# Eight of the fourteen slots of the second MLP's down-layer weights combined beside the first MLP

## The chip, the cores and the metric

The kernel runs on one core of a Trainium2 chip. The metric is the device time of one execution in microseconds, the median of several runs. The engines are named as in the profile: PE is TensorE, PEld its weight loads, DVE is VectorE, ACT is ScalarE, POOL is GpSimd and SP is SyncE, which issues all DMAs of this kernel.

## The reference

A linear attention with an RMS norm gives x of 8 batches, 576 tokens and 512 features. Two blocks follow, each with an MLP of 2048 hidden features:

```python
X = np.fft.fft(np.fft.fft(x, axis=1), axis=2)
u = x + np.real(X)
un = (u - mu) / np.sqrt(var + 1e-06)
x = u + np.maximum(un @ w_ch1, 0.0) @ w_ch2          # first MLP, weights moe_*

u = x + ((x.transpose(0, 2, 1) @ U) @ V).transpose(0, 2, 1)
out = u + np.maximum(u @ w_ch1, 0.0) @ w_ch2         # second MLP, weights moe2_*
```

All is fp32, and the kernel must keep nearly all of that precision.

## The kernel before

**Stages.** Attention and the Fourier transform take the first 280 us. Then come 12 rounds (`g` in the code, `NG`), each of 768 tokens: rounds 0 to 5 are the first MLP, rounds 6 to 11 (`g >= NS`, `NS` = 6) the second. Each layer is a Strassen product: the 2 x 2 blocks of tokens and weights are combined into 7 products (1 to 7), for which sums or differences of blocks are needed on both sides. Each operand is split into a high and a low part (fp32r), and PE computes high*high, high*low and low*high.

**Steps.** A round has 56 steps (`t`), 28 of the up layer (lines L838 to L840) and 28 of the down layer (L855 to L857), each of 12 matmuls of 384 columns. "Down half" is steps 28 to 55. The down products go in the order `DN_ORDER` = (2, 5, 1, 4, 3, 7, 6), four steps each. For each down step DVE makes the low part `t_lo` (`lo_dn`, L1332), and for products of two blocks it or, for every fourth step, POOL first adds the blocks of h (`raw_dn`: L1351 on DVE, L1556 on POOL); ACT makes the high part (`hi_dn`, L1068 and L1074). There are five buffers of these entries, so an entry is made at most five steps ahead. DVE also takes finished products out of PSUM: `d5` (L1377) at its place 36, `d1` (L1381) at 40, and so on. In the second MLP, after `d1`, POOL adds a block twice (`add_first`, L1566).

**Weights.** Two steps share a slot of weights, so a round has 28 slots (14 up, 14 down) that go through a ring of 7 buffers of 1 MB (`RING`). A slot is either loaded ready, combined and split, from the scratch tensors `wc1` and `wc2` (L515), or made from the raw weights ("raw slot"): SP loads one or two blocks (L509), POOL adds them if there are two (`sum_slot`, L1542, 8 steps ahead of the use), ACT makes the high part (`split_slot_hi`, L987, 7 ahead), DVE the low part (`split_slot_lo`, L1266, 6 ahead), and SP stores the result to `wc2` for the rounds that follow (`store_w`, L526). In rounds 0 and 6 all 14 down slots are raw. Products 3 and 4 take one block and need no sum.

**Up pieces.** The combined up weights of the second MLP are made in rounds 1 to 4 already: eight units go through the buffer `pb_v`, two in a round: load at step 2 or 30, five small sums on POOL 4 steps later, ACT 7 later, DVE 8 later (L1260), and two stores.

**Orders by hand.** Each engine walks through all rounds and steps in a fixed order, with semaphore waits; what is listed at step t runs when the engine gets there. Rounds 1 to 6 have, between the steps of the up half, the turning of the last round's result (PE L722), its sum (DVE L1405) and split (`split_x2_lo`, DVE L1410, which writes `x_lo`), and a gather product (PE L752 to L754, at steps 4, 7, ..., 19) that waits for `x_lo`. Rounds 5 and 6 mix the second block's input in (L764, DVE L1421).

Of the kernel before, what the change touches and what calls it, by code (L numbers as in the profile page):

```python
# [166 lines left out]
def build_program(nc, k_main, k_rest, v_main, v_rest, q_t, g_norm, wr1a, wr2a, wr1b, wr2b, u_perm, v_perm,  # L169
# [114 lines left out]
    with ExitStack() as ctx:  # L284
# [12 lines left out]
        def sem(name):  # L297
# [38 lines left out]
        PB = {"0": (pb[0], pb_raw[0]), "1": (pb[1], pb_raw[1]), "v": (pb_v, pb_v_raw)}  # L336
        UNITS = [("01"[f % 2], f // 2, 0, f) for f in range(8)] + [("v", f, 1, f) for f in range(8)]
        UNIT_AT = {(1 + f // 2, 2 + 28 * (f % 2)): UNITS[8 + f] for f in range(8)}

        def stored_units(mlp, h):  # L340

# [3 lines left out]
                    need[name] = max(need.get(name, 0), n + 1)  # L345
            return need

        def slot_sum(r, i):

            high, low = w_raw[r][:, 0, :, :, :], w_raw[r][:, 1, :, :, :]  # L350
# [47 lines left out]
        def _(sp):  # L398
# [9 lines left out]
            def load_unit(unit):  # L408
                name, n, mlp, f = unit
                if n:  # L410
                    sp.wait_ge(p_stored[name], 32 * n)
                sp.dma_start(PB[name][1][:, 0, 0:4, :], wr[mlp][0][:, f // 4, :, f % 4].rearrange("b p c -> p b c")).then_inc(
                    p_loaded[name], 16)

            def store_unit(unit):
                name, n, mlp, f = unit
                sp.wait_ge(p_lo[name], n + 1)
                for part in range(2):
                    sp.dma_start(wc1[mlp][:, f // 4, :, part, f % 4].rearrange("i p c -> p i c"),
                                 PB[name][0][:, part, :, :].bitcast(F32)).then_inc(p_stored[name], 16)  # L420
# [68 lines left out]
            def load_w(n):  # L489

                r, mlp = n % RING, n // NSLOT // NS
                layer = n % NSLOT // len(UP_SLOTS)
                i, h = slot_product(n)
                if n >= RING:

                    sp.wait_ge(step, 2 * (n - RING) + 2)
                    if stored_slot(n - RING):
                        sp.wait_ge(w_stored[r], 16 * stores_of(n - RING))
                if raw_slot(n):
                    blocks = wr[mlp][layer][:, h].rearrange("b p f c -> b p (f c)")  # L500
                    names = {1: (0, 3), 2: (2, 3), 3: (0,), 4: (3,), 5: (0, 1), 6: (0, 2), 7: (1, 3)}[i]
# [59 lines left out]
            for g in range(NG):  # L561
                for j in range(NSLOT):
# [354 lines left out]
        def _(act):  # L917
# [56 lines left out]
            def split_unit_hi(unit):  # L974
# [169 lines left out]
            for g in range(NG):  # L1144
                more = g < NG - 1
                for t in range(NSTEP):
# [42 lines left out]
                            deviation(3 * (g + 1) + LN_AT.index(t - 1))  # L1189
                    if (g, t - 7) in UNIT_AT:  # L1190
                        split_unit_hi(UNIT_AT[g, t - 7])
                    for n in RAW_SLOTS:
                        if NSTEP * g + t == max(0, 2 * n - 7):
                            split_slot_hi(n)

        @block.vector
        def _(dve):
# [237 lines left out]
            for g in range(NG):  # L1435
                more = g < NG - 1
                for t in range(NSTEP):
# [65 lines left out]
        def _(pool):  # L1503
# [21 lines left out]
            def sum_unit(unit):  # L1525
# [8 lines left out]
                nc.gpsimd.tensor_tensor(raw[:, 1, 3, :], a21, a11, ALU.subtract)  # L1534
                nc.gpsimd.tensor_tensor(raw[:, 1, 4, :], a12, a22, ALU.subtract).then_inc(p_summed[name], 1)

            def sum_slot(n):

                r = n % RING
                pool.wait_ge(w_loaded[r], 16 * (n // RING + 1))  # L1540
                x, y, op = slot_sum(r, slot_product(n)[0])
# [46 lines left out]
            for g in range(NG):  # L1588
                more = g < NG - 1
                for t in range(NSTEP):  # L1590
# [94 lines left out]
```

## Time and profile before

| | |
|---|---|
| median of 3 runs | 1872.03 us (1871.91 to 1872.23) |
| the profiled execution | 1872.23 us, of which 1869.9 us from first to last instruction |
| granted TensorE clock, mean | 0.973 |
| PE busy | 1758.9 us, 94% |
| DVE busy | 1376.1 us, 74% |
| ACT busy | 783.4 us, 42% |
| POOL busy | 601.4 us, 32% |
| DMA | 470.04 MB, 251 GB/s on the mean |

A stretch in which PE's busy time falls behind the stretch's length is one where something else sets the time; which one is read from the wait before its matmuls. The bounds of the stretches below are the first up and down matmuls of the rounds: round 3's down half begins at 762.2 us, round 5 at 951.4, its down half at 1020.2, round 6 at 1082.3, its down half at 1153.1, round 7 at 1233.6 and its down half at 1299.9.

### The profile page before, as it was taken

What the parts mean: (1) busy time and instruction counts of PE and PEld (TensorE: products, weight loads), DVE (VectorE), ACT (ScalarE), POOL (GpSimd) and SP (SyncE); (2) the same over time, 40 slices, a digit from 0 to 9 for tenths busy, and PEclk for the clock granted to TensorE, in tenths of its full rate; (3) what the DMA queues carried; (4) which work ended last, traced back from release to release, by engine and by line L of the source; (5) the groups of instructions that cost most, each with busy time, mean ns of one, the idle gap of its engine ahead of it and who ended that gap; (6) DMA issues with size and microseconds to landing.
All of it is one profiled execution on the core that took longest, in us unless ns stands there. A gap on an engine that the chain in (4) does not pass through costs nothing.

```text
span 1869.9 us, 25843 instructions
## 1 busy us (share of the span) xinstructions
PE 1758.9 (94%) x9908; PEld 1691.3 (90%) x9908; DVE 1376.1 (74%) x1559; ACT 783.4 (42%) x1126; POOL 601.4 (32%) x428
## 2 busy tenths in 40 slices
PE   5989878889999999999999999799999999999998
PEld 5777758879999999999999999789999999999998
DVE  4787875997786787777866768965856947758667
ACT  1333333634544544444444436334335434443442
POOL 2777873453042131240320213620410402303203
PEclk9989879989999999999999999899999999999999
DMA  7457548888788688787876678786766666766663
GB/s 250 160 200 233 189 163 295 304 325 308 254 293 287 247 286 286 264 301 256 296 261 239 241 252 308 284 306 221 240 240 240 233 240 248 248 222 238 229 248 121
DMA packets 123819, 470.04 MB, mean 251 GB/s; under 512 B 12273, under 2 KB 49649, under 8 KB 84018
## 3 DMA queue, kind: packets, MB, share of 16 engines
q1 hardware_dynamic: 123698, 468.39, 71.5%
q8 instruction: 81, 1.33, 0.3%
q14 instruction: 40, 0.33, 0.1%
HBM read 389.70 MB, written 78.64 MB: 250 GB/s over the span
## 4 chain that ended last, share of the span: by engine, by line
PE 71%; DVE 11%; POOL 8%; issue 5%; DMA 3%; SPq 1%; ACT 0%; DVEq 0%; POOLq 0%; ACTq 0%
PE pair L838 11%; PE pair L840 11%; PE pair L839 11%; PE pair L855 11%; PE pair L857 10%; PE pair L856 10%; DVE t_raw L1351 3%; DVE t_lo L1332 2%; PE tr_ps L722 2%; DMA in_sb<-x_dram 1%; POOL x_sb L1520 1%; POOL x_sb L1511 1%; DMA q_sb<-q_t 1%; POOL w_raw L1542 1%; POOL x_sb L1519 1%
## 5 line engine op out<-in xcount | busy, mean ns | idle before, releaser
L855 PE MATMUL pair<-t_hi,w_sb 128*128 128x384 f32 x1344 | 463.1, 345 | 32.1 <-DVE t_lo L1332 31.9
L838 PE MATMUL pair<-t_hi,w_sb 128*128 128x384 f32 x1344 | 460.8, 343 | 17.3 <-DVE h_sb L1369 9.2
L856 PE MATMUL pair<-t_lo,w_sb 128*128 128x384 f32 x1344 | 458.8, 341 | 0.0
L857 PE MATMUL pair<-t_hi,w_sb 128*128 128x384 f32 x1344 | 458.5, 341 | 0.0
L839 PE MATMUL pair<-t_lo,w_sb 128*128 128x384 f32 x1344 | 455.8, 339 | 0.0
L840 PE MATMUL pair<-t_hi,w_sb 128*128 128x384 f32 x1344 | 455.6, 339 | 0.0
L1332 DVE TENSOR_TENSOR t_lo<-t_raw,t_hi 128x768 fp32r<-128x768 f32 x300 | 349.0, 1171 | 17.1 <-ACT t_hi L1059 13.7
L1556 POOL TENSOR_TENSOR t_raw<-h_sb 128x768 f32<-128x768 f32 x60 | 150.3, 2504 | 574.1 <-PE pair L857 574.1
L1074 ACT ACTIVATE t_hi<-t_raw 128x768 fp32r<-128x768 f32 x240 | 202.1, 846 | 314.2 <-DVE t_raw L1351 236.1
L855 PEld LDWEIGHTS pair<-t_hi,w_sb 128*128 128x128 f32 x1344 | 255.0, 190 | 41.1 <-DVE t_lo L1332 40.8
L838 PEld LDWEIGHTS pair<-t_hi,w_sb 128*128 128x128 f32 x1344 | 252.8, 188 | 24.5 <-issue 19.7
L839 PEld LDWEIGHTS pair<-t_lo,w_sb 128*128 128x128 f32 x1344 | 252.9, 188 | 3.0
L856 PEld LDWEIGHTS pair<-t_lo,w_sb 128*128 128x128 f32 x1344 | 255.0, 190 | 0.3
L857 PEld LDWEIGHTS pair<-t_hi,w_sb 128*128 128x128 f32 x1344 | 255.0, 190 | 0.0
L840 PEld LDWEIGHTS pair<-t_hi,w_sb 128*128 128x128 f32 x1344 | 252.8, 188 | 0.0
L1556 POOL TENSOR_TENSOR t_raw<-a_sb 128x768 f32<-128x768 f32 x60 | 124.9, 2085 | 322.6 <-PE pair L840 283.8
L1351 DVE TENSOR_TENSOR t_raw<-h_sb 128x768 f32<-128x768 f32 x180 | 206.4, 1147 | 20.0 <-PE pair L857 20.0
L1332 DVE TENSOR_TENSOR t_lo<-h_sb,t_hi 128x768 fp32r<-128x768 f32 x96 | 96.3, 1016 | 23.4 <-ACT t_hi L1068 23.4
L1266 DVE TENSOR_TENSOR w_sb<-w_raw,w_sb 128x1024 fp32r<-128x1024 f32 x76 | 109.7, 1443 | 0.6 <-ACT w_sb L987 0.6
L1373 DVE TENSOR_TENSOR h_sb<-pair,h_sb 128x768 f32<-128x768 f32 x48 | 46.0, 958 | 84.7 <-PE pair L840 84.6
L1511 POOL TENSOR_TENSOR x_sb<-x_sb,gn_sb 96x256 f32<-96x256 f32 x96 | 78.2, 845 | 84.1 <-DVE x_sb L1214 84.1
L1364 DVE TENSOR_TENSOR h_sb<-pair,h_sb 128x768 f32<-128x768 f32 x48 | 46.0, 958 | 68.3 <-PE pair L840 68.3
(149 smaller groups left out, 2120.9 us busy)
## 6 DMA issues: line engine op xcount, KB each, us to landing
w_sb<-wc SPq DMA_DIRECT2D x260, 1024.0 KB, 4.9
wc<-w_sb SPq DMA_DIRECT2D x28, 1024.0 KB, 5.5
w_raw<-wr1a SPq DMA_DIRECT2D x24, 512.0 KB, 5.0
w_raw<-wr1b SPq DMA_DIRECT2D x24, 512.0 KB, 4.3
wc<-pb SPq DMA_DIRECT2D x16, 640.0 KB, 4.8
w_raw<-wr2a SPq DMA_DIRECT2D x10, 1024.0 KB, 7.0
wc<-pb_v SPq DMA_DIRECT2D x16, 640.0 KB, 4.8
w_raw<-wr2b SPq DMA_DIRECT2D x10, 1024.0 KB, 6.4
```

What stands on the lines that cost most here:

```text
L838: nc.tensor.matmul(ps, w_hi, hi[:, x, :], start=(fresh and x == 0), stop=False, skip_group_check=True)
L839: nc.tensor.matmul(ps, w_hi, lo[:, x, :], start=False, stop=False, skip_group_check=True)
L840: last = nc.tensor.matmul(ps, w_lo, hi[:, x, :], start=False, stop=(x == 1), skip_group_check=True)
L855: nc.tensor.matmul(ps, w_hi, hi[:, f, :], start=(fresh and k == 0 and f == 0), stop=False, skip_group_check=True)
L856: nc.tensor.matmul(ps, w_hi, lo[:, f, :], start=False, stop=False, skip_group_check=True)
L857: last = nc.tensor.matmul(ps, w_lo, hi[:, f, :], start=False, stop=(k == 3 and f == 1), skip_group_check=True)
L1074: nc.scalar.activation(t_hi[r][:, :, :], t_raw[r][:, :, :], ACT.Copy).then_inc(hi_ready, 1)
L1266: nc.vector.tensor_tensor(w_sb[r][:, 1, :, :, :], w_raw[r][:, 1, :, :, :], w_sb[r][:, 0, :, :, :].bitcast(F32), ALU.subtract).then_inc(w_l ...
L1332: nc.vector.tensor_tensor(t_lo[r][:, :, :], src, t_hi[r][:, :, :].bitcast(F32), ALU.subtract).then_inc(lo_ready, 1)
L1351: nc.vector.tensor_tensor(t_raw[(NENT * g + e) % ENT_RING][:, :, :], x, y, op).then_inc(raw_dve, 1)
L1511: last = nc.gpsimd.tensor_tensor(x, x, gn_sb[:, :].unsqueeze(1).to_broadcast([PT, H // 2, HD]), ALU.mult)
L1556: nc.gpsimd.tensor_tensor(t_raw[r][:, :, :], x, y, op).then_inc(raw_pool, 1)
```

## The change

The down slots of products 5, 1, 7 and 6 of the second MLP (two halves each, eight slots) are no longer raw in round 6. Eight jobs make them in rounds 1 to 4, two in a round, in a tile at the place of `pb_v`: SP loads two blocks (1 MB) at step 16 or 44, POOL adds them at 20 or 48, ACT makes the high part at 23 or 51, DVE the low part at 24 or 52, and SP stores 1 MB to `wc2`. Each job waits until the unit before it is stored, and each unit until the job before it is. Round 6 loads these eight slots ready. Its slots of products 2, 4 and 3 (six) stay raw.

```diff
 STORED = (1, 2, 5, 6, 7)
+AHEAD = (5, 1, 7, 6)
@@ def raw_slot(n):
-    return UP_SLOTS[j][0] not in STORED if j < len(UP_SLOTS) else g % NS == 0
+    if j < len(UP_SLOTS):
+        return UP_SLOTS[j][0] not in STORED
+    return g == 0 or g == NS and DN_SLOTS[j - len(UP_SLOTS)][0] not in AHEAD
...
+        JOBS = [(i, h) for i in AHEAD for h in range(2)]
+        JOB_AT = {(1 + x // 2, 16 + 28 * (x % 2)): x for x in range(len(JOBS))}
@@ SP
+                if n and mlp:
+                    sp.wait_ge(job_stored, 16 * n)                    # load_unit
...
+            def load_job(x):
+                sp.wait_ge(p_stored["v"], 32 * (x + 1))
+                sp.dma_start(job_raw..., wr2b[a:b + 1:b - a, h]...).then_inc(job_loaded, 16)
+            def store_job(x):
+                sp.wait_ge(job_lo, x + 1)
+                sp.dma_start(wc2[1][i - 1, h]..., job_sb...).then_inc(job_stored, 16)
...
+                    if (g, t) in JOB_AT:
+                        load_job(JOB_AT[g, t])
+                    if (g, t - 8) in JOB_AT:
+                        store_job(JOB_AT[g, t - 8])
...
+                if layer == 1 and n // NSLOT == NS:
+                    sp.wait_ge(job_stored, 16 * len(JOBS))            # load_w
@@ ACT, at step t - 7
+                act.wait_ge(job_summed, x + 1)
+                nc.scalar.activation(job_sb[:, 0, :, :, :], job_raw[:, 1, :, :, :], ACT.Copy).then_inc(job_hi, 1)
@@ DVE, at step t - 8
+                dve.wait_ge(job_hi, x + 1)
+                nc.vector.tensor_tensor(job_sb[:, 1, :, :, :], job_raw[:, 1, :, :, :], job_sb[:, 0, :, :, :].bitcast(F32),
+                                        ALU.subtract).then_inc(job_lo, 1)
@@ DVE, round NS - 1, step 0, before the memset of vp_raw
+                        dve.wait_ge(job_stored, 16 * len(JOBS))
@@ POOL, at step t - 4
+                pool.wait_ge(job_loaded, 16 * (x + 1))
+                a, b, op = slot_sum(job_raw, JOBS[x][0])
+                nc.gpsimd.tensor_tensor(job_raw[:, 1, :, :, :], a, b, op).then_inc(job_summed, 1)
```

## Rows read from the trace of the kernel before

**Rows 1.** The page: busy time, share of the span and instructions of TensorE.
```profile
PE 1758.9 (94%) x9908; PEld 1691.3 (90%) x9908; DVE 1376.1 (74%) x1559; ACT 783.4 (42%) x1126; POOL 601.4 (32%) x428
```

**Rows 2.** Stretches: length, busy us of PE, PEld, DVE, ACT, POOL; PEclk, DMA share, GB/s.
```profile
762.20:822.40 60.20, 60.20 (x345) 60.13 (x344) 51.61 (x50) 28.68 (x35) 23.65 (x13) 1.00 0.82 289
951.40:1020.20 68.80, 68.80 (x398) 66.76 (x397) 42.99 (x51) 30.30 (x41) 4.16 (x3) 1.00 0.72 245
1020.20:1082.30 62.10, 62.10 (x357) 61.73 (x355) 47.27 (x49) 28.16 (x36) 15.50 (x8) 1.00 0.70 252
1082.30:1153.10 70.80, 69.13 (x397) 66.64 (x397) 46.47 (x51) 33.13 (x44) 16.79 (x8) 1.00 0.75 253
1153.10:1233.60 80.50, 67.36 (x358) 64.58 (x357) 79.44 (x63) 35.78 (x44) 41.87 (x15) 0.94 0.85 322
1299.90:1361.40 61.50, 59.91 (x338) 59.26 (x337) 52.16 (x48) 25.03 (x30) 23.29 (x10) 1.00 0.71 240
```

**Rows 3.** The trace in order of time, PE, round 6: start, us, instruction [idle before].
```profile
1195.14 0.69 PE L855 MATMUL pair<-t_hi,w_sb 128*128 128x384 f32 x1 [5.52 <-DVE t_lo L1332]
```

**Rows 4.** Groups by line and shape: count | busy us, mean ns | idle before.
```profile
L1542 POOL TENSOR_TENSOR w_raw<-w_raw 128x1024 f32<-128x1024 f32 x20 | 59.0, 2953 | 66.1 <-DMA w_raw<-wr2a 36.4 <-DMA w_raw<-wr2b 29.7
```

**Rows 5.** The trace in order of time, DVE and POOL, round 6.
```profile
1138.31 1.83 DVE L1332 TENSOR_TENSOR t_lo<-h_sb,t_hi 128x768 fp32r<-128x768 f32 x1
1156.50 4.03 DVE L1332 TENSOR_TENSOR t_lo<-h_sb,t_hi 128x768 fp32r<-128x768 f32 x2
...
1169.64 3.27 POOL L1556 TENSOR_TENSOR t_raw<-h_sb 128x768 f32<-128x768 f32 x1 [10.80 <-PE pair L857]
```

**Rows 6.** The trace in order of time, DVE, round 5.
```profile
1038.76 0.96 DVE L1377 TENSOR_TENSOR ch_sb<-ch_sb,pair 128x768 f32<-128x768 f32 x1 [2.28 <-PE pair L857]
...
1048.14 0.96 DVE L1381 TENSOR_TENSOR ch_sb<-pair,ch_sb 128x768 f32<-128x768 f32 x1 [1.75 <-PE pair L857]
```

**Rows 7.** The trace in order of time around step 19, round 3.
```profile
732.44 5.69 SPq L515 DMA_DIRECT2D w_sb<-wc  x2
740.77 1.22 DVE L1266 TENSOR_TENSOR w_sb<-w_raw,w_sb 128x1024 fp32r<-128x1024 f32 x1
741.91 0.68 DVE L1410 TENSOR_TENSOR x_lo<-res_sb,x_hi 128x512 fp32r<-128x512 f32 x1
...
743.19 0.39 PE L752 MATMUL gt_ps<-x_hi,up_hi 128*64 128x512 f32 x1
```

**Rows 8.** The trace in order of time, DVE, rounds 7 and 6.
```profile
1325.52 0.96 DVE L1381 TENSOR_TENSOR ch_sb<-pair,ch_sb 128x768 f32<-128x768 f32 x1 [1.45 <-PE pair L857]
...
1327.26 2.60 DVE L1351 TENSOR_TENSOR t_raw<-h_sb 128x768 f32<-128x768 f32 x1
1329.79 2.60 DVE L1332 TENSOR_TENSOR t_lo<-t_raw,t_hi 128x768 fp32r<-128x768 f32 x1
...
1189.24 2.84 DVE L1266 TENSOR_TENSOR w_sb<-w_raw,w_sb 128x1024 fp32r<-128x1024 f32 x1
```

**Rows 9.** The trace in order of time around step 19, round 6 (POOL, DVE).
```profile
1127.20 2.41 POOL L1542 TENSOR_TENSOR w_raw<-w_raw 128x1024 f32<-128x1024 f32 x1 [13.49 <-DMA w_raw<-wr2b]
1127.60 0.95 DVE L1369 TENSOR_TENSOR h_sb<-h_sb,pair 128x768 f32<-128x768 f32 x1
...
1129.06 1.63 DVE L1266 TENSOR_TENSOR w_sb<-w_raw,w_sb 128x1024 fp32r<-128x1024 f32 x1
```

**Rows 10.** The page's DMA issues: count, KB each, median us to landing.
```profile
wc<-w_sb SPq DMA_DIRECT2D x28, 1024.0 KB, 5.5
...
w_raw<-wr2a SPq DMA_DIRECT2D x10, 1024.0 KB, 7.0
...
w_raw<-wr2b SPq DMA_DIRECT2D x10, 1024.0 KB, 6.4
```

**Rows 11.** The trace in order of time, DVE, end of round 3.
```profile
814.12 0.96 DVE L1399 TENSOR_TENSOR ch_sb<-pair,ch_sb 128x768 f32<-128x768 f32 x1 [2.29 <-PE pair L857]
815.00 3.64 DVE L1332 TENSOR_TENSOR t_lo<-t_raw,t_hi 128x768 fp32r<-128x768 f32 x3
```

More of the change, by code:

```diff
@@ L228, in build_program @@
     pb_v_raw = at("pb_v_raw", a0 + 69632, [128, 2, 5, 256])
+    job_sb = at("job_sb", a0 + 69632, [128, 2, 4, 2, 128], F32R)
+    job_raw = at("job_raw", a0 + 69632, [128, 2, 4, 2, 128])
     c0 = a0 + 81248
@@ L331, in build_program @@
         up_zeroed, up_loaded, up_split_hi, up_split_lo = sem("up_zeroed"), sem("up_loaded"), sem("up_split_hi"), sem("up_split_lo")
+        job_loaded, job_summed, job_hi = sem("job_loaded"), sem("job_summed"), sem("job_hi")
+        job_lo, job_stored = sem("job_lo"), sem("job_stored")
         vp_zeroed, vp_loaded, vp_split_hi, vp_split_lo = sem("vp_zeroed"), sem("vp_loaded"), sem("vp_split_hi"), sem("vp_split_lo")
@@ L346, in stored_units, with slot_sum @@
             return need
-        def slot_sum(r, i):
-            high, low = w_raw[r][:, 0, :, :, :], w_raw[r][:, 1, :, :, :]
+        def slot_sum(raw, i):
+            high, low = raw[:, 0, :, :, :], raw[:, 1, :, :, :]
             return {1: (high, low, ALU.add), 2: (high, low, ALU.add), 5: (high, low, ALU.add),
@@ L420, in store_unit @@
                                  PB[name][0][:, part, :, :].bitcast(F32)).then_inc(p_stored[name], 16)
+            def load_job(x):
+                i, h = JOBS[x]
+                a, b = BLOCKS[i]
+                sp.wait_ge(p_stored["v"], 32 * (x + 1))
+                sp.dma_start(job_raw[:, :, :, :, :].rearrange("p l f x c -> p l (f x c)"),
+                             wr2b[a:b + 1:b - a, h].rearrange("b p f c -> b p (f c)").rearrange("b p c -> p b c")).then_inc(
+                                 job_loaded, 16)
+            def store_job(x):
+                i, h = JOBS[x]
+                sp.wait_ge(job_lo, x + 1)
+                sp.dma_start(wc2[1][i - 1, h].rearrange("p l f c -> p (l f c)"),
+                             job_sb[:, :, :, :, :].rearrange("p l f x c -> p (l f x c)").bitcast(F32)).then_inc(job_stored, 16)
             for n in range(2):
@@ L500, in load_w @@
                     blocks = wr[mlp][layer][:, h].rearrange("b p f c -> b p (f c)")
-                    names = {1: (0, 3), 2: (2, 3), 3: (0,), 4: (3,), 5: (0, 1), 6: (0, 2), 7: (1, 3)}[i]
+                    names = BLOCKS[i]
                     if len(names) == 1:
@@ L978, in split_unit_hi, with split_job_hi @@
                 nc.scalar.activation(p[:, 0, :, :], raw[:, 1, :, :], ACT.Copy).then_inc(p_hi[name], 1)
+            def split_job_hi(x):
+                act.wait_ge(job_summed, x + 1)
+                nc.scalar.activation(job_sb[:, 0, :, :, :], job_raw[:, 1, :, :, :], ACT.Copy).then_inc(job_hi, 1)
             def split_slot_hi(n):
@@ L1191, in _ @@
                         split_unit_hi(UNIT_AT[g, t - 7])
+                    if (g, t - 7) in JOB_AT:
+                        split_job_hi(JOB_AT[g, t - 7])
                     for n in RAW_SLOTS:
@@ L1496, in _ @@
                         split_unit_lo(UNIT_AT[g, t - 8])
+                    if (g, t - 8) in JOB_AT:
+                        split_job_lo(JOB_AT[g, t - 8])
                     for n in RAW_SLOTS:
@@ L1535, in sum_unit, with sum_job @@
                 nc.gpsimd.tensor_tensor(raw[:, 1, 4, :], a12, a22, ALU.subtract).then_inc(p_summed[name], 1)
+            def sum_job(x):
+                pool.wait_ge(job_loaded, 16 * (x + 1))
+                a, b, op = slot_sum(job_raw, JOBS[x][0])
+                nc.gpsimd.tensor_tensor(job_raw[:, 1, :, :, :], a, b, op).then_inc(job_summed, 1)
             def sum_slot(n):
@@ L1540, in sum_slot @@
                 pool.wait_ge(w_loaded[r], 16 * (n // RING + 1))
-                x, y, op = slot_sum(r, slot_product(n)[0])
+                x, y, op = slot_sum(w_raw[r], slot_product(n)[0])
                 nc.gpsimd.tensor_tensor(w_raw[r][:, 1, :, :, :], x, y, op).then_inc(w_summed, 1)
@@ L1607, in _ @@
                         sum_unit(UNIT_AT[g, t - 4])
+                    if (g, t - 4) in JOB_AT:
+                        sum_job(JOB_AT[g, t - 4])
                     for n in RAW_SLOTS:
```

2 lines of the change are left out of this document (added).

## The prediction, made before the change was run

> **What bounds the kernel now.** The first view is the page's busy time: PE works for 94% of the span [rows 1], so a change pays only where PE waits. The second is the busy time by stretch, cut at the bounds of the rounds' halves; the reader compares halves with the same PE work. Round 5's down half and round 6's down half both hold the mixing of the second block, yet the one takes 62.1 us and the other 80.5: 18.4 us more. In the first DVE is busy for 47.3 us, in the second for 79.4 of 80.5, without a pause. The up halves take 68.8 and 70.8 us: 2.0 us more [rows 2]. So round 6 holds 20.4 us in which PE waits or runs at the lower clock. Round 7's down half, which has no raw down slot, still takes 61.5 us against 60.2 in round 3, although it has no turning of inputs in it: a wait of its own is left (below). The third view, the trace in order of time, names what ends the longest wait: 5.52 us until DVE's `t_lo` [rows 3]. DVE is the bound of that half; its load is the low parts and block sums, plus 14 splits (L1266), plus the time for which POOL keeps it out.
>
> **What the change takes from round 6.** Eight POOL sums (20 sums of both MLPs take 2.95 us each on the mean [rows 4]), eight ACT copies, eight DVE splits, eight stores and half the loaded bytes' combining. POOL's sums matter by what they do to DVE. A `t_lo` takes 0.95 us alone (two in a row 1.82); beside a sum one took 1.83, and two beside another took 4.03, so 2.2 us were lost. POOL can lose too: an addition that arrived in a run of DVE operations took 3.27 us [rows 5].
>
> Up half: the 1.83 us stood beside the sum of product 5's first slot, which goes; DVE reaches the reading of PSUM for which PE waits 0.9 us earlier. Slot 14 (product 2) stays raw, and with it the other 1.1 us. Gain 0.9.
>
> Down half: what stays are the splits of slots 20, 21, 22, 23 (products 4 and 3), at steps 34, 36, 38, 40. I put them into round 5's half, which has all the rest. There DVE stands idle for 2.28 us before `d5` and 1.75 us before `d1` [rows 6]. One split costs 1.14 us from start to start (740.77 to 741.91 in round 3 [rows 7]). Slot 20's fits into the 2.28; slots 21 and 22 need 2.28 against 1.75, so DVE leaves `d1` 0.5 us late, or 1.8 if POOL's addition for step 39 costs it a turn (up to 1.65, below). After `d1` comes what round 7 has too: two POOL additions, each of which holds one DVE operation to 2.60 us, 1.65 more than 0.95; PE waits there already in round 7 (about 2.1 us in all, which is how its 61.5 us come about). In round 6 slot 23's split stands in this row as well, 1.14 us more. So the step that waits is late by 0.8 (round 7's share at this step) + 1.14 + 0.5 to 1.8, and the next by 1.1 to 1.3 as in round 7 [rows 8]: 3.5 to 5.0 us in all, against 18.4. I take 4.0, near the lower end, since the other addition (step 35) meets DVE's idle time. The later waits of the half, around steps 51 and 52, came with the splits and sums of product 6 and go. Gain 14.4, with bounds 11 and 16.3 (18.4 less round 7's 2.1). The clock is a part of it: it was granted at 0.94 over the old half [rows 2], after a wait of 5.5 us, and at the lower of its levels (1.2 instead of 2.4 GHz) a step, 60.2 / 28 = 2.15 us, takes as much again. Round 7 kept 1.00 with 2.1 us of waits; mine lie between the two, so one step at the lower clock, some 2 us, is in the upper bound of the remainder (7 us, hence the 11). Round 6 in all: 15.3 us less.
>
> **What it adds to rounds 1 to 4.** Per round two POOL sums of 2.4 us or more, two ACT copies of 1 us, two DVE splits of 1.14, 4 MB of transfers. PE is busy there through the whole down half (60.20 of 60.20 us [rows 2]), so any wait is paid in full.
>
> Jobs at step 16 (four). In round 6, a sum at 1127.20 stood in the same place, before step 19. DVE's reading of PSUM beside it (0.95) was not held, but the split of a weight slot (L1266) was: 1.63 instead of 1.22, until 1.1 us after the sum's end [rows 9]. In round 3 this split starts at 740.77, `x_lo` follows at 741.91 and ends at 742.59, and PE's gather, which waits for it, starts at 743.19, so there is 0.6 us to spare [rows 7]. The job's load is issued right behind the slot's load of 732.44, at about 732.9. Such loads of two blocks land 6.4 to 7.0 us after issue [rows 10]; behind a full slot I take 7.0. The sum then runs from 739.9 to 742.3, before the split can start, the split ends at 743.4, `x_lo` at 744.1, and the gather starts 1.0 us late. With 6.4 us it would be 0.3 to 0.4; with a landing just before 740.77 it is 1.7; after that the split comes first and nothing is lost. I take 1.0 each, 4.0 for four; ends 0 and 6.8.
>
> Jobs at step 44 (four). The load stands behind a slot and two residuals and lands around step 48; the sum falls into DVE's run of steps 48 to 51. DVE has one pause there, 2.29 us before `d7`, and then three low parts in a row, 3.64 us, one of them held by POOL's additions for the last steps and the next round [rows 11]. Sum and split take 1.65 to 2.2 + 1.14 = 2.8 to 3.3 us from a pause of 2.29, and POOL's additions are pushed behind them; its first one for the next round is needed by step 0. I take the difference, 0.5 to 1.0: 0.7 each, 2.8 for four. The ends: 0, since the low parts are up to two steps (4 us) ahead, and a turn of 1.65 each, 6.6.
>
> At nothing: ACT's copies, for it is busy 28.7 of 60.2 us; the bytes, 4 MB in 129 us or 33 GB/s on top of 289, where round 6 carried 322 [rows 2]; SP's queue, where the next slot's load waits for PE's step anyway, and slots are loaded 12 steps (25 us) ahead, so even one that lands 5 us later is in time. POOL does nothing else between steps 12 and 35 but the unit's sums. The splits at step 24 meet a DVE pause. The new wait of DVE at round 5, step 0, for the last store: issued by about step 54, landing in 5.5 us [rows 10], it comes at step 0 or 1, when DVE arrives. Behind it stand the memset and low parts not due before step 6; uncovered it could cost 2 us once.
>
> **Sum.** 15.3 - 4.0 - 2.8 = 8.5 us. The profiled execution took 1872.23 us (span 1869.9), 0.2 above the median: 1872.0 - 8.5 = 1863.5 us.
>
> One rule speaks against this change. The rows show that POOL and DVE hold each other up, and also that DVE's runs may keep POOL out (3.27 us). The Trainium skill, "SBUF — State Buffer", section "Who interferes with whom", says that a DVE instruction with two SBUF inputs contends with a GpSimd instruction that reads SBUF, and its section on the two sides adds that whoever starts first holds the shared port for its whole instruction. By that rule the step-16 jobs lose their time as worked out, which the 1.63 us bear out, and the sums of the step-44 jobs cost a full turn; that is the third rival.
>
> **The rivals.**
> *The jobs are free.* If the loads at step 16 land after 740.8 and the low parts' lead covers step 48, only round 6 is left: 1872.0 - 15.3 = 1856.7. For it: the units' five sums run at step 34 of these rounds, and PE's down half has no wait. Against: the numbers at step 19.
> *The six slots that stay keep DVE full.* They are the ones before the old wait's place. If POOL's additions at steps 35 and 39 each cost a turn before `d1` and the clock falls, the remainder is 5.0 + 1.65 + 2 = 9 to 10 instead of 4: 1863.5 + 5.5 = 1869. Against: round 5's idle time of 4.0 us.
> *Every lock in full.* Step 16 at 1.7 and step 44 at 1.65 cost 13.4 instead of 6.8: 1870.1, no change or nearly.
> *The other side: slower.* If POOL's sums and DVE's splits of the jobs come to stand wholly in PE's way, each costs 2.2 + 1.14 = 3.3 us, eight 26.7, and the kernel takes 1872.0 - 15.3 + 26.7 = 1883.4. It decides from 15.3 / 8 = 1.9 us a job on. DVE's pauses, 2.29 us before `d7`, are against it.
>
> **How the numbers follow.** My forecast 0.43 (its own range 1861 to 1866.5), free jobs 0.25, six slots 0.12, every lock 0.12, slower 0.05, the rest 0.03. The range takes the first four but for their far edges: 1856 to 1869.5. About 0.2% (3.7 us) can be told from no change: same is what falls between 1868.3 and 1875.8, most of the two rivals near 1869 and 1870 (0.14 of the chance), slower 0.06, faster 0.80.
>
> **What the profile will show.** Round 6's down half: some 66 us, not 80.5, clock near 1.00, and a wait for `t_lo` around steps 42 to 44 alone. Its up half 69.9. In rounds 1 to 4: L1266 before step 19 over 2 us and PE's gather 1 us late, up halves 69.8; down halves up by 0.7 or the next round's first step late. The forecast is wrong if the up halves stay at 68.8 (the load landed elsewhere), if the jobs' sums stretch to over 4 us (POOL waits, not DVE), or if round 6 still waits before `d1`.

## The result, and the profile after

| | before | after |
|---|---|---|
| median | 1871.84 us (6 runs, 1866.17 to 1872.23) | 1877.47 us (6 runs, 1875.04 to 1881.38) |
| profiled execution, its span | 1872.23, 1869.9 us | 1875.04, 1872.8 us |
| granted TensorE clock, mean | 0.973 | 0.974 |

The ratio is 1.0037, with a 95% interval of 1.0021 to 1.0053: the change made the kernel slower, by 5.6 us between the medians (6.9 between the means, which the ratio goes by). The forecast was 1863.5, faster. The two profiled executions lie 2.8 us apart: that of after was its fastest run, that of before its slowest. The halves below account for that difference, and the other 2.8 us between the medians can be read in no trace.

The busy time by stretch of the kernel after answers to [rows 2]. The columns are the same (the length of the stretch, then the busy us of PE, PEld, DVE, ACT and POOL); the stretches are round 2's down half, round 3's halves, round 5's halves and round 6's halves.

```profile
638.00:702.50 64.50, 61.52 (x346) 59.72 (x345) 59.21 (x51) 30.26 (x37) 28.84 (x14) 1.00 0.82 302
702.50:771.30 68.80, 68.13 (x394) 66.12 (x395) 51.99 (x69) 31.98 (x45) 11.23 (x8) 1.00 0.86 298
771.30:834.50 63.20, 60.98 (x346) 59.94 (x344) 58.05 (x51) 30.24 (x37) 27.82 (x14) 1.00 0.84 309
...
967.40:1036.30 68.90, 68.90 (x396) 66.78 (x397) 43.58 (x52) 29.43 (x40) 3.70 (x2) 1.00 0.72 249
1036.30:1098.40 62.10, 62.10 (x357) 61.72 (x356) 47.32 (x49) 28.21 (x36) 15.46 (x8) 1.00 0.70 250
1098.40:1168.20 69.80, 69.03 (x399) 66.78 (x397) 44.05 (x51) 31.28 (x42) 9.01 (x5) 1.00 0.76 257
1168.20:1236.60 68.40, 63.89 (x357) 63.19 (x356) 57.65 (x55) 30.60 (x38) 22.26 (x10) 0.98 0.73 257
```

From first matmul to first matmul of the halves:

| | before | after | difference |
|---|---|---|---|
| start of the rounds | 280.2 | 281.3 | +1.1 |
| round 0 | 155.0 | 154.2 | -0.9 |
| up halves of rounds 1, 2, 3, 4 | 68.8 each | 69.6, 69.8, 68.9, 69.7 | +2.8 |
| down halves of rounds 1, 2, 3, 4 | 60.2 each | 63.1, 64.5, 63.2, 63.2 | +13.0 |
| round 5's halves | 68.8, 62.1 | 68.9, 62.1 | +0.2 |
| round 6's up half | 70.8 | 69.8 | -1.1 |
| round 6's down half | 80.5 | 68.4 | -12.0 |

Nothing is changed ahead of round 1; the start of the rounds lay between 278.8 and 282.0 us in all kernels of this study, and round 0 took 153.0 to 156.1, so the first two lines say nothing. Round 6 gives 13.1 us, where I forecast 15.3. The up halves cost 2.8, forecast 4.0. The down halves cost 13.0, forecast 2.8: here the gain went.

**Where a down half loses 3 us.** The trace in order of time of the kernel after, DVE, end of round 3, answers to [rows 11]. The added code has moved the lines: DVE's `t_lo` is L1381 now (L1332 before), its `t_raw` L1400 (L1351), POOL's additions L1613 (L1556), and PE's down steps begin at L893 (L855).

```profile
815.75 0.95 DVE L1400 TENSOR_TENSOR t_raw<-h_sb 128x768 f32<-128x768 f32 x1
816.62 3.16 DVE L1381 TENSOR_TENSOR t_lo<-t_raw,t_hi 128x768 fp32r<-128x768 f32 x1
...
821.44 2.60 DVE L1400 TENSOR_TENSOR t_raw<-h_sb 128x768 f32<-128x768 f32 x1
823.95 2.60 DVE L1381 TENSOR_TENSOR t_lo<-t_raw,t_hi 128x768 fp32r<-128x768 f32 x1
826.47 0.94 DVE L1448 TENSOR_TENSOR ch_sb<-pair,ch_sb 128x768 f32<-128x768 f32 x1
827.34 0.94 DVE L1381 TENSOR_TENSOR t_lo<-t_raw,t_hi 128x768 fp32r<-128x768 f32 x1
828.21 1.21 DVE L1309 TENSOR_TENSOR job_sb<-job_raw,job_sb 128x1024 fp32r<-128x1024 f32 x1
829.34 5.11 DVE L1381 TENSOR_TENSOR t_lo<-t_raw,t_hi 128x768 fp32r<-128x768 f32 x2
```

The same stretch on POOL:

```profile
816.14 2.81 POOL L1592 TENSOR_TENSOR job_raw<-job_raw 128x1024 f32<-128x1024 f32 x1 [1.13 <-DMA job_raw<-wr2b]
821.23 1.98 POOL L1613 TENSOR_TENSOR t_raw<-h_sb 128x768 f32<-128x768 f32 x1 [2.27 <-PE pair L895]
823.42 2.32 POOL L1613 TENSOR_TENSOR t_raw<-a_sb 128x768 f32<-128x768 f32 x1 [0.21 <-PE pair L895]
829.14 4.50 POOL L1613 TENSOR_TENSOR t_raw<-a_sb 128x768 f32<-128x768 f32 x2 [3.40 <-PE pair L895]
```

And on PE, where the wait before step 53 is paid; a second one, of 0.89 us, follows before step 55:

```profile
826.60 0.45 PE L893 MATMUL pair<-t_hi,w_sb 128*128 128x384 f32 x1 [1.21 <-DVE t_lo L1381]
```

Before, only two of POOL's four additions met a busy DVE. The first ran in DVE's pause ahead of `d7`. The second ran beside the reading of `d7` and held the low part behind it by 0.95 us (the 3.64 us for three in [rows 11]). The third held one low part to 2.59 us, 1.65 more. The fourth ran mostly in a second pause, of 1.45 us. These are the POOL rows of the kernel before, and its DVE behind [rows 11]:

```profile
812.05 1.84 POOL L1556 TENSOR_TENSOR t_raw<-h_sb 128x768 f32<-128x768 f32 x1 [6.24 <-PE pair L857]
814.23 1.85 POOL L1556 TENSOR_TENSOR t_raw<-a_sb 128x768 f32<-128x768 f32 x1 [0.34 <-PE pair L857]
818.47 1.86 POOL L1556 TENSOR_TENSOR t_raw<-a_sb 128x768 f32<-128x768 f32 x1 [2.39 <-PE pair L857]
820.59 2.27 POOL L1556 TENSOR_TENSOR t_raw<-a_sb 128x768 f32<-128x768 f32 x1 [0.26 <-PE pair L857]
```
```profile
818.56 2.59 DVE L1332 TENSOR_TENSOR t_lo<-a_sb,t_hi 128x768 fp32r<-128x768 f32 x1
822.60 0.96 DVE L1399 TENSOR_TENSOR ch_sb<-pair,ch_sb 128x768 f32<-128x768 f32 x1 [1.45 <-PE pair L857]
```

After, POOL's sum at 816.14 holds a `t_lo` to 3.16 us, 2.2 more than 0.95. DVE then reaches `d7` (826.47) without a pause, 3.2 us later in the half than before. The additions, which PE's progress lets go at the same steps as before, now all find DVE busy, and each holds one operation: 2.60, 2.60, and 5.11 for two. So the four additions hold DVE for 4 × 1.65 = 6.6 us, where before they held it for 0.95 + 1.65 = 2.6. DVE's work from the row at 815.75 to the reading of `d6` just behind the half grows by 7.2 us: some 4.0 by the additions, 2.2 by the job's sum and 1.1 by the split. The two pauses, 2.29 and 1.45, took up 3.7 of it; some 3.5 us are left, and the half is 2.9 longer. In round 2 the job's sum starts directly behind one of POOL's additions, and that half loses 4.2.

**The jobs at step 16.** The same view of the kernel after, round 1, DVE and then PE:

```profile
482.88 2.52 DVE L1315 TENSOR_TENSOR w_sb<-w_raw,w_sb 128x1024 fp32r<-128x1024 f32 x1
485.32 0.68 DVE L1459 TENSOR_TENSOR x_lo<-res_sb,x_hi 128x512 fp32r<-128x512 f32 x1
```
```profile
486.06 0.45 PE L790 MATMUL gt_ps<-x_hi,up_hi 128*64 128x512 f32 x1 [0.60 <-DVE x_lo L1459]
```

The sum (481.94, 2.38 us) holds the slot's split to 2.52 us instead of 1.22 [rows 7], `x_lo` comes later, and the gather waits, as worked out. In round 3 the load landed later, and the sum began at 751.52, behind `x_lo`; PE waited for nothing.

**Round 6's down half**, the view of waits (the engine and what it waits for: us in total, times, longest):

```profile
PE pair L893 <- DVE t_lo L1381: 4.5, 1, 4.5
```

The one wait that is left is where it was expected, before step 43.

### The profile page after: what moved, and what is told of

Its sections match the earlier page's. It is cut to its first block, busy times and chain, and to the rows that moved or that the text cites. A ratio compares the mean times of both kernels' runs of the same rounds, so it can differ in the third digit from the quotient of the medians.

```text
span 1872.8 us, 25858 instructions
## 1 busy us (share of the span) xinstructions
PE 1754.1 (94%) x9908; PEld 1686.0 (90%) x9908; DVE 1389.5 (74%) x1559; ACT 783.7 (42%) x1126; POOL 593.9 (32%) x428
## 3 DMA queue, kind: packets, MB, share of 16 engines
q8 instruction: 81, 1.33, 0.3%
## 4 chain that ended last, share of the span: by engine, by line
PE 66%; DVE 15%; POOL 8%; issue 7%; DMA 2%; SPq 1%; ACT 1%; DVEq 0%; POOLq 0%; ACTq 0%
PE pair L876 11%; PE pair L878 11%; PE pair L877 11%; PE pair L893 9%; PE pair L895 9%; PE pair L894 9%; DVE t_lo L1381 5%; DVE t_raw L1400 3%; PE tr_ps L760 2%; POOL x_sb L1572 2%; POOL x_sb L1563 1%; DMA in_sb<-x_dram 1%; DMA q_sb<-q_t 1%; POOL x_sb L1571 1%; POOL x_sb L1573 1%
## 5 line engine op out<-in xcount | busy, mean ns | idle before, releaser
L893 PE MATMUL pair<-t_hi,w_sb 128*128 128x384 f32 x1344 | 462.3, 344 | 32.9 <-DVE t_lo L1381 32.9
L1381 DVE TENSOR_TENSOR t_lo<-t_raw,t_hi 128x768 fp32r<-128x768 f32 x300 | 363.7, 1218 | 17.0 <-ACT t_hi L1101 13.6
L1613 POOL TENSOR_TENSOR t_raw<-h_sb 128x768 f32<-128x768 f32 x60 | 148.9, 2482 | 593.9 <-PE pair L895 593.9
L893 PEld LDWEIGHTS pair<-t_hi,w_sb 128*128 128x128 f32 x1344 | 254.5, 189 | 41.0 <-DVE t_lo L1381 40.7
L1613 POOL TENSOR_TENSOR t_raw<-a_sb 128x768 f32<-128x768 f32 x60 | 124.8, 2083 | 337.0 <-PE pair L878 292.6
L1400 DVE TENSOR_TENSOR t_raw<-h_sb 128x768 f32<-128x768 f32 x180 | 206.4, 1147 | 22.0 <-PE pair L895 22.0
L1381 DVE TENSOR_TENSOR t_lo<-h_sb,t_hi 128x768 fp32r<-128x768 f32 x96 | 92.0, 970 | 25.5 <-ACT t_hi L1110 25.5
L1413 DVE TENSOR_TENSOR h_sb<-pair,h_sb 128x768 f32<-128x768 f32 x48 | 46.0, 958 | 68.4 <-PE pair L878 68.4
```

The lines of the kernel that those rows point to most:

```text
L893: nc.tensor.matmul(ps, w_hi, hi[:, f, :], start=(fresh and k == 0 and f == 0), stop=False, skip_group_check=True)
L1381: nc.vector.tensor_tensor(t_lo[r][:, :, :], src, t_hi[r][:, :, :].bitcast(F32), ALU.subtract).then_inc(lo_ready, 1)
L1400: nc.vector.tensor_tensor(t_raw[(NENT * g + e) % ENT_RING][:, :, :], x, y, op).then_inc(raw_dve, 1)
L1613: nc.gpsimd.tensor_tensor(t_raw[r][:, :, :], x, y, op).then_inc(raw_pool, 1)
```

## The experiments

All ratios and "before" medians are from the same chip as the run beside them. A median without an interval is of one run.

| kernel | us | before | ratio (95%) | up halves 1 to 4, more | down halves 1 to 4, more | round 6 |
|---|---|---|---|---|---|---|
| after | 1877.47 | 1871.84 | 1.0037 (1.0021 to 1.0053) | 2.8 | 13.0 | 69.8 + 68.4 |
| no late sum | 1862.98 | 1871.89 | | 5.3 | 0.3 | 69.8 + 68.4 |
| no late split on DVE | 1875.33 | 1871.51 | | 6.1 | 8.6 | 69.8 + 69.5 |
| early jobs only | 1875.25 | 1871.89 | 1.0018 (1.0008 to 1.0027) | 2.7 | 0 | 69.8 + 80.4 |
| late sums on DVE | 1863.67 | 1871.89 | 0.9959 (0.9943 to 0.9975) | 3.9 | 0.3 | 69.8 + 68.4 |
| late jobs only, on DVE | 1861.05 | 1871.51 | 0.9949 (0.9932 to 0.9965) | 0.2 | 0 | 70.8 + 68.5 |
| early jobs two steps later | 1862.46 | 1871.51 | 0.9954 (0.9939 to 0.9968) | 1.2 | 3.1 | 69.8 + 68.5 |
| no sums on POOL | 1855.67 | 1871.51 | 0.9922 (0.9907 to 0.9936) | 0.2 | 0.4 | 70.8 + 63.8 |
| late sum as a fill | 1868.54 | 1871.75 | | 6.1 | 0 | 70.3 + 68.9 |
| no sums on POOL, zeroes later | 1856.17 | 1871.75 | 0.9917 (0.9899 to 0.9935) | 0.0 | 0 | 70.9 + 63.8 |

"Early" are the jobs of step 16, "late" those of step 44; "no sums on POOL" means no sum of a job. The kernels without the late sum, without the late split and with the fill leave out part of the late jobs' weights, so their output is not the reference's.

### 1. POOL's sum of the late jobs left out

```diff
             def split_job_hi(x):
-                act.wait_ge(job_summed, x + 1)
+                if x % 2:
+                    act.wait_ge(job_loaded, 16 * (x + 1))
+                else:
+                    act.wait_ge(job_summed, x // 2 + 1)
@@ POOL
-                    if (g, t - 4) in JOB_AT:
+                    if (g, t - 4) in JOB_AT and JOB_AT[g, t - 4] % 2 == 0:
```

> As the changed kernel, but POOL's sum is left out of the four jobs of step 44 (the raw block is split instead, so the output is not the reference's); load, ACT copy, DVE split and store stay. The turn theory (POOL's sum holds one DVE operation for 2.2 us, the pause of 2.29 us is gone, and POOL's later additions then each hold a DVE operation): the down halves of rounds 1, 3, 4 fall from 63.1 to 63.2 us back to 60.2 to 60.6. The rival that DVE's 1.14 us split at step 52 is what is too much: they stay above 62. The rival that the added traffic is at fault: they stay at 63.1.

The down halves of rounds 1, 3 and 4 are back at 60.2 us, round 2's at 60.6, although ACT's copy, DVE's split and both transfers are still there. The window of round 3:

```profile
765.10:825.30 60.20, 60.20 (x345) 60.13 (x345) 52.92 (x51) 29.58 (x36) 23.91 (x13) 1.00 0.86 316
```

DMA moves 316 GB/s there, more than in the slower half of after (309), so traffic isn't the cause; nor are ACT and SP. DVE is busy 52.9 us: 1.3 more than before, the split.

### 2. DVE's split of the late jobs left out

For a first form of this test, with the split cut to 1 column of 128, there is no result; its expectation is on record:

> As the changed kernel, but in the four jobs of step 44 DVE's low part covers 1 of 128 columns in each block (about 0.1 us instead of 1.2; the rest of the low part is left out, so the output is not the reference's). POOL's sum stays. The turn theory: most of the 2.9 us a down half stay, about 1.1 go (62.0 us). The split rival: all goes (60.2). The traffic rival: nothing goes (63.1).

In its place ACT fills the low part with a second copy:

```diff
                 nc.scalar.activation(job_sb[:, 0, :, :, :], job_raw[:, 1, :, :, :], ACT.Copy).then_inc(job_hi, 1)
+                if x % 2:
+                    act.wait_ge(job_hi, x + 1)
+                    nc.scalar.activation(job_sb[:, 1, ...], job_sb[:, 0, ...].bitcast(F32), ACT.Copy).then_inc(job_lo, 1)
@@ DVE
-                    if (g, t - 8) in JOB_AT:
+                    if (g, t - 8) in JOB_AT and JOB_AT[g, t - 8] % 2 == 0:
```

> As the changed kernel, but in the four jobs of step 44 DVE's split is left out: ACT fills the low part's place with a second copy, so those weights' low parts are wrong and the output is not the reference's. POOL's sum stays. The turn theory: the sum alone starts it, so of the 2.9 us that each of the down halves of rounds 1, 3 and 4 lost, 1.1 go with the split and 1.8 stay (62.0 us). If sum and split were only too much together (the split-and-sum rival), all goes (60.2).

```profile
772.30:834.00 61.70, 60.49 (x345) 60.09 (x345) 56.13 (x50) 29.96 (x37) 27.25 (x14) 1.00 0.86 320
```

With the sum alone a down half (here round 3's) takes 61.7: 1.5 us more than before. With the split alone it was 0, with both 2.9. The two prices don't add up: they draw on the same pauses, and only what goes beyond these reaches PE. Without the split DVE still has a pause of 0.73 us ahead of its reading at 834.22; without the sum it has the whole 2.28 ahead of `d7`. In round 2, where the sum stands right behind one of POOL's additions, it costs 4.2 us by itself, as much as both.

### 3. The early jobs alone

Products 5 and 1 only, their four jobs at step 16 of rounds 1 to 4; products 7 and 6 are raw in round 6 again.

```diff
-AHEAD = (5, 1, 7, 6)
+AHEAD = (5, 1)
-        JOB_AT = {(1 + x // 2, 16 + 28 * (x % 2)): x for x in range(len(JOBS))}
+        JOB_AT = {(1 + x, 16): x for x in range(len(JOBS))}
```

> Four jobs alone, those of step 16 (products 5 and 1, rounds 1 to 4); products 7 and 6 are combined in round 6 again. Down halves of rounds 1 to 4 back to 60.2 us if the step-44 jobs alone cost the 13 us; up halves of 69.6 to 69.8 as in the changed kernel in most rounds. Round 6's down half between 68.4 and 80.5: POOL's four sums and four splits of products 7 and 6 return, and they are what stood at steps 43 to 52, so I expect 75. Sum: 3 us lost early, 5.5 + 1 won in round 6: 1 to 5 us faster than before. If the sums of products 5 and 1 had been the ones that filled DVE, it would be 68 to 70 and the kernel 8 to 10 us faster.

This expectation failed for round 6, and with it for the time: 3.4 us slower by the medians, where 1 to 5 us faster was expected. The window is round 6's down half:

```profile
1153.50:1233.90 80.40, 67.33 (x357) 64.50 (x356) 73.65 (x59) 33.65 (x42) 38.35 (x14) 0.94 0.74 270
```

The down half is as long as before (80.5), although DVE has 5.8 us less to do in it, and its four longest waits are those of the kernel before to within 0.05 us (1.45, 5.52, 1.33 and 2.68 us before steps 41, 43, 44 and 45). The work of products 5 and 1 comes early in the half, where DVE has time; what makes the wait stands at steps 40 to 44, and is that of products 7 and 6. POOL and DVE there:

```profile
1179.41 1.85 POOL L1613 TENSOR_TENSOR t_raw<-h_sb 128x768 f32<-128x768 f32 x1 [6.75 <-PE pair L895]
1181.22 3.36 POOL L1599 TENSOR_TENSOR w_raw<-w_raw 128x1024 f32<-128x1024 f32 x1
```
```profile
1182.27 3.13 DVE L1381 TENSOR_TENSOR t_lo<-t_raw,t_hi 128x768 fp32r<-128x768 f32 x1
```

All that products 5 and 1 give is 1.1 us of the up half, for 2.7 paid in rounds 1 to 4: they make the kernel slower by themselves.

### 4. The late sums on DVE

ACT's copy one step later, split and store two; the sum is in DVE's order at step 51, ahead of `d7`.

```diff
+            def sum_job_dve(x):
+                dve.wait_ge(job_loaded, 16 * (x + 1))
+                a, b, op = slot_sum(job_raw, JOBS[x][0])
+                nc.vector.tensor_tensor(job_raw[:, 1, :, :, :], a, b, op).then_inc(job_summed_dve, 1)
@@ DVE
+                    if (g, t - 7) in JOB_AT and JOB_AT[g, t - 7] % 2:
+                        sum_job_dve(JOB_AT[g, t - 7])
```

> All eight jobs; in the four of step 44 the sum is made by DVE (1.14 us, in its pause at step 51) instead of POOL, ACT copies at step 52, DVE splits at 54. DVE gets 1.14 us more work, POOL 2.4 less. The turn theory: down halves of rounds 1 to 4 at 60.2 to 61.0, the kernel 9 to 12 us faster than before. The theory that DVE's work itself is too much there: over 63.1, slower than the changed kernel.

```profile
818.75 1.21 DVE L1312 TENSOR_TENSOR job_raw<-job_raw 128x1024 f32<-128x1024 f32 x1
821.10 0.96 DVE L1455 TENSOR_TENSOR ch_sb<-pair,ch_sb 128x768 f32<-128x768 f32 x1 [1.14 <-PE pair L896]
```

The same sum takes 1.2 us on DVE instead of 2.8 on POOL with 2.2 lost on DVE. It lies in the pause, and 1.14 us of this is left, for POOL's next addition. The down halves are at 60.2 to 60.5 again with the whole work done: 0.9959, a faster kernel, by 8.2 us between the medians where 9 to 12 were expected; the up halves take 3.9 us more, 1.1 above those of the changed kernel.

### 5. The late jobs alone, summed on DVE

Experiment 4 with `AHEAD = (7, 6)` and `JOB_AT = {(1 + x, 44): x ...}`.

> Four jobs alone, products 7 and 6, one in each of rounds 1 to 4, all of step 44 with the sum on DVE; products 5 and 1 are combined in round 6 as before. If, as the run with products 5 and 1 alone suggests, all of round 6's gain comes from products 7 and 6: round 6's down half 68.4 us, its up half 70.8, rounds 1 to 4 as before (68.8 and 60.2), the kernel 11 to 13 us faster than before. The rival that each of the eight slots gives its share: 74 us and 6 us faster.

```profile
951.20:1021.00 69.80, 69.06 (x398) 66.71 (x397) 46.25 (x52) 30.50 (x42) 5.54 (x3) 1.00 0.76 258
1153.90:1222.40 68.50, 63.95 (x358) 63.25 (x356) 63.43 (x59) 32.65 (x40) 25.97 (x11) 0.98 0.87 318
```

Round 6's down half is 68.5, as with all eight slots moved: its whole gain of 12.0 us comes from four slots. Together with experiment 3 this settles it from both sides. Round 5's up half (first row) is 1.0 us longer: DVE waits 1.94 us for the last store ahead of its memset, `x_lo` then runs beside an operation of POOL (2.34 us instead of 0.68), and the gather behind step 4 waits for it. The kernel is 10.5 us faster by the medians, just under the 11 to 13 expected.

### 6. The early jobs two steps later

Experiment 4 with the early jobs at step 18 instead of 16.

> All eight jobs, late sums on DVE, and the early jobs two steps later (load at 18, sum on POOL at 22, ACT 25, DVE 26), so that the sum comes after the low part that PE's gather waits for. Up halves of rounds 1 to 4 back to 68.8 us (they were 68.8 to 70.5 with the load at 16), all else as with the sums on DVE: 2 to 4 us faster than that kernel, 11 to 13 than before. The rival, that a sum anywhere in the up half costs PE 1 us: no difference to the kernel with the load at 16.

The up halves of rounds 1, 2 and 4 are back at 68.8 to 68.9 (round 3's is 69.8). But the later store of the job delays the unit behind it. In round 3 its five sums push POOL's next addition 2.3 us later in the half, to 780.70, and this one and the one at 786.52 each hold an operation of DVE (the rows below): the down halves get 0.2 to 1.3 us longer. In round 5 DVE waits 2.64 us for the last store. So the waits moved rather than went; 1862.46 here against experiment 4's 1863.67 can't be told apart.

```profile
780.99 2.38 DVE L1388 TENSOR_TENSOR t_lo<-t_raw,t_hi 128x768 fp32r<-128x768 f32 x1
...
786.76 2.60 DVE L1407 TENSOR_TENSOR t_raw<-h_sb 128x768 f32<-128x768 f32 x1
```

### 7. No job's sum on POOL

Products 4 and 3 (one block, no sum) at step 16, products 7 and 6 at step 44 with the sum on DVE. Products 2, 5 and 1 stay raw, so their sums are still POOL's in round 6.

```diff
-AHEAD = (5, 1, 7, 6)
+AHEAD = (4, 7, 3, 6)
-        JOBS = [(i, h) for i in AHEAD for h in range(2)]
+        JOBS = [(i, h) for pair in ((4, 7), (3, 6)) for h in range(2) for i in pair]
@@ load_job
+                if x % 2 == 0:
+                    sp.dma_start(job_raw[:, 1, ...], wr2b[a, h]...).then_inc(job_loaded, 16)
+                    return
```

> Eight jobs, but of products 4 and 3 (one block, no sum) at step 16 and of 7 and 6 at step 44 with the sum on DVE; products 2, 5 and 1 stay raw in round 6. No sum of a job is on POOL. Rounds 1 to 4: 68.8 and 60.2 us. Round 6's down half loses the splits of slots 20 to 23 too; slot 23's 1.14 and the lateness before it go: 64 to 66 us if DVE's work between steps 34 and 42 sets it, 68.4 if only POOL's additions there do. Up half 70.8. The kernel 14 to 17 us faster than before in the first case, 11 to 12 in the second.

The window is round 6's down half:

```profile
1153.40:1217.20 63.80, 62.63 (x357) 61.60 (x355) 59.23 (x54) 28.52 (x36) 28.12 (x12) 1.00 0.83 309
```

As many jobs, chosen by where their work stood, give 0.9922: 15.8 us by the medians. Rounds 1 to 4 lose 0.6 us in all, and round 6's down half falls to 63.8, since `d1` now comes after an idle 1.75 us, and only POOL's two additions behind it and the one after them hold DVE, as in round 7 [rows 8]. Against experiment 5 the splits of products 4 and 3 were worth 4.6 us:

```profile
1181.37 0.96 DVE L1444 TENSOR_TENSOR ch_sb<-pair,ch_sb 128x768 f32<-128x768 f32 x1 [1.75 <-PE pair L900]
1182.25 0.95 DVE L1395 TENSOR_TENSOR t_lo<-t_raw,t_hi 128x768 fp32r<-128x768 f32 x1
1183.11 2.60 DVE L1414 TENSOR_TENSOR t_raw<-h_sb 128x768 f32<-128x768 f32 x1
1185.64 2.61 DVE L1395 TENSOR_TENSOR t_lo<-t_raw,t_hi 128x768 fp32r<-128x768 f32 x1
```

### 8. POOL's sum replaced by a fill of like length

```diff
+                if x % 2:
+                    nc.gpsimd.memset(job_raw[:, :, :, :, :], 0.0).then_inc(job_summed, 1)
+                    return
                 nc.gpsimd.tensor_tensor(job_raw[:, 1, :, :, :], a, b, op).then_inc(job_summed, 1)
```

> As the changed kernel, but in the four jobs of step 44 POOL fills the tile with zeroes instead of adding (it writes 2048 columns and reads nothing, so those weights are wrong and the output is not the reference's). POOL is busy at the same place, for 1 to 2 us. If it is the reading of two operands on POOL that holds DVE (turn theory), the down halves of rounds 1 to 4 are 60.2 us and DVE's low parts beside the fill take 0.95. If POOL's time as such, which pushes its next additions, is what costs, they stay at 62 to 63.

POOL, then DVE beside it, end of round 3:

```profile
814.38 1.81 POOL L1593 MEMSET job_raw<- 128x2048 f32 x1 [1.08 <-DMA job_raw<-wr2b]
```
```profile
814.04 0.95 DVE L1400 TENSOR_TENSOR t_raw<-h_sb 128x768 f32<-128x768 f32 x1
814.91 0.94 DVE L1381 TENSOR_TENSOR t_lo<-t_raw,t_hi 128x768 fp32r<-128x768 f32 x1
815.77 0.94 DVE L1400 TENSOR_TENSOR t_raw<-h_sb 128x768 f32<-128x768 f32 x1
...
821.62 0.96 DVE L1448 TENSOR_TENSOR ch_sb<-pair,ch_sb 128x768 f32<-128x768 f32 x1 [2.29 <-PE pair L895]
```

POOL is busy for 1.81 us at the same place (a sum takes 2.38 alone) and waits for the same load, but holds nothing, the pause before `d7` is whole, and the down halves are 60.2. So it is POOL's reading and adding beside DVE that costs, not the new wait in its queue. Nor does POOL's time push its next addition: in the kernel after, POOL stood idle for 2.27 us between the sum and the addition at 821.23.

### 9. The zeroes of round 5 four steps later

Experiment 7 with the wait for the last store and the memset behind it at step 4 instead of 0, and the loads, ACT's copy and the split that follow from it 3 to 4 steps later.

> As the kernel without sums on POOL, and the zeroing of the tile that follows the jobs' tile is moved from round 5, step 0, to step 4 (its loads from 2 to 6, ACT's copy from 8 to 11, DVE's split from 9 to 12). DVE no longer waits for the last job's store at step 0. Round 5's up half from 69.6 back to 68.8 us, nothing else: 0.8 us faster than that kernel, 16 to 17 than before. If the 0.8 us were not this wait, no change.

The wait at step 4 is gone, but the split of `vp_lo`, now at step 12, runs beside POOL's addition there, pushes `x_lo`, and the gather waits 1.3 us:

```profile
981.36 2.31 DVE L1540 TENSOR_TENSOR vp_lo<-vp_raw,vp_hi 128x1152 fp32r<-128x1152 f32 x1
```

The expectation failed: round 5's up half is 70.2, not 68.8, and there is no gain over experiment 7; the two times can't be told apart.

## Why the prediction was wrong

**The step that failed** is "Jobs at step 44 (four)": "I take the difference, 0.5 to 1.0: 0.7 each", with the ends "0" and "a turn of 1.65 each". Measured: 13.0 for four, 3.2 each, beyond the upper end. I counted the turn that the job's own sum takes and wrote that "POOL's additions are pushed behind them", but gave that no price. Before, these four additions held DVE for 2.6 us, since two of them ran in its pauses; with the pauses gone each of them cost a turn of its own, 6.6 us in all. Experiment 1 shows that the sum is necessary for the loss, experiment 2 that it makes 8.6 of the 13.0 alone, experiment 8 that a POOL operation in the same place which reads nothing costs nothing there, experiment 4 that the loss goes when the same sum is DVE's. That the four additions carry the rest is read from the rows at 821 to 834 us beside those of before; no run took them away by themselves.

**The rival on the other side** had the mechanism of these jobs: sums and splits wholly in PE's way, 3.3 us each. Its price was met by the four late jobs (3.2 each), not by the early ones, so its 1883.4 was too high. That the price fits is luck: the split by itself cost nothing and the sum by itself 1.5 us (experiments 1 and 2), not 1.14 and 2.2 in PE's way, and 4.0 us came from additions that this rival doesn't count, with the pauses taking up 3.7. Its deciding point of 1.9 us a job was nearly what happened: (13.0 + 2.8) / 8 = 2.0 us a job, against a gain of 13.1 / 8 = 1.6. I had given it 0.05 on the ground of the pause of 2.29 us; that pause was spoken for.

**Other rivals.** Free jobs: no, they cost 15.8 us. The six slots that stay: their remainder is 6.3, not 9 to 10; its own terms, 5.0 + 1.65 + 2, add up to 8.65, and its time to 1868.2, not 1869. Every lock in full: right in that the late sums cost full turns, but it counted one turn a job where the rows show more.

**Jobs at step 16**: right. 0.8, 1.0 and 0.9 in rounds 1, 2 and 4, by the mechanism told, with loads that landed 6.9 to 7.0 us after issue, as I had put in. In round 3 the load took 9.5 us and landed behind the start of `x_lo`, and nothing was lost, a case I had named. Where it lands varies: other kernels with the same jobs lost 0.1 to 1.8 a round. The late jobs' loads took 8.4 to 8.5 us.

**Round 6, up half**: 0.9 forecast, 1.1 measured.

**Round 6, down half**: right in kind, 2.4 us too much. I took a remainder of 4.0 (bounds 2.1 to 7); it is 68.4 - 62.1 = 6.3: the one wait of 4.5, inside the 3.5 to 5.0 that I had for the waits, and 1.8 by which PE is busy longer (63.89 against 62.10). These 1.8 us are in the main the step at the lower clock, which I had put into the bound alone: behind the wait, from 1207.4 to 1212.0 us, the granted clock was 0.63, that is, partly at 1.2 instead of 2.4 GHz. DVE's rows show where the wait comes from. The split of slot 22 ran beside POOL's addition for step 39 and took 2.42 us, and `d1` was read at 1197.83, 1.5 us behind the start of step 40 (1196.33) where round 7 has 0.2: 1.3 late, between my 0.5 and 1.8. Behind it three operations, not two, are held before the low part of step 43 is ready; in round 7 the third of them comes behind that low part, and PE pays for it before step 44 instead:

```profile
1194.62 2.42 DVE L1315 TENSOR_TENSOR w_sb<-w_raw,w_sb 128x1024 fp32r<-128x1024 f32 x1
1196.96 0.95 DVE L1381 TENSOR_TENSOR t_lo<-t_raw,t_hi 128x768 fp32r<-128x768 f32 x1
1197.83 0.94 DVE L1430 TENSOR_TENSOR ch_sb<-pair,ch_sb 128x768 f32<-128x768 f32 x1
...
1199.56 2.59 DVE L1400 TENSOR_TENSOR t_raw<-h_sb 128x768 f32<-128x768 f32 x1
1202.08 2.84 DVE L1315 TENSOR_TENSOR w_sb<-w_raw,w_sb 128x1024 fp32r<-128x1024 f32 x1
1204.84 2.55 DVE L1381 TENSOR_TENSOR t_lo<-t_raw,t_hi 128x768 fp32r<-128x768 f32 x1
```

What I had not seen at all is whose work the 14.4 us were: I charged it to eight slots, and experiments 3 and 5 show that in the down half four of them gave everything and four nothing.

**At nothing**: the traffic, ACT and SP's queue cost nothing (experiment 1: 316 GB/s and 60.2 us). Round 5's wait was covered in the kernel after (0.2 us) and in experiment 4 (0.1), and cost 1.0, 1.9 and 0.8 in experiments 5, 6 and 7, whose last store landed later in the round.

**By the forecast's own terms**: up halves -1.2 us against it, round 6 +2.2, late jobs +10.2; 8.5 us of gain less 11.2 gives 2.7 us slower, the 2.8 of the profiled pair.

**What stays open**: the other 2.8 us between the medians. Runs of after spread over 6.3 us, and only the fastest has a trace; of before, only the slowest.

## What to carry to other kernels

Price work that is moved into a stretch by the pauses that it fills, and list who fills them already: a second engine's operations that ran in a pause each cost a turn once it is gone, so here two additions that had been free cost 3.3 us together (1.65 each). Before moving eight pieces out of a full stretch, ask which of them stand ahead of the wait that ends last; here four carried all of the down half's gain, and the other four cost more than they gave. Where an addition on POOL holds DVE, as in these rows, the shorter of the two forms (1.2 us on DVE in a pause against 2.8 on POOL with 2.2 lost) is worth more than an even load.

## What the runs showed of the hardware

POOL's sum held a one-input operation of DVE too. In the kernel after, round 3, two of them in a row took 2.90 us beside the sum at 751.52, where the same two took 1.00 in the kernel before. I had counted only the operations with two inputs.

```profile
751.89 2.90 DVE L1372 TENSOR_SCALAR in_sb<-in_sb,mv_sb,ri_sb 128x512 f32<-128x512 f32 x2
```

The Trainium skill, "SBUF — State Buffer", section "Who interferes with whom", lets operations of this kind enter a mode in which they contend with GpSimd; the trace agrees, with 1.9 us lost. By its rule for operations with two SBUF inputs only a GpSimd operation that reads SBUF is in the way; the fill of experiment 8, with DVE at 0.94 to 0.95 us beside it, agrees too.

An operation of POOL that meets a busy DVE does not have one price. In [rows 5] one waited 1.4 us itself (3.27 instead of some 1.85); in the kernel after, 4.50 us for two on POOL went with 5.11 for two on DVE, each taking turns with the other.
